# An attention and two feed-forward layers on one core: the order of softmax steps, key sums and weight splits in the front is changed

## The reference

```python
# q, k, v: (4, 8, 576, 64); factor = 4; scale = 1 / sqrt(64)
q_d, k_d, v_d = (mean of 4 neighbouring positions of q, k, v)      # 144 positions
out_d = softmax(scale * q_d @ k_d.T) @ v_d                         # "group" attention
out_up = np.repeat(out_d, 4, axis=2)
mask = np.abs(pos[:, None] - pos[None, :]) < 4                     # "local" attention
out_local = softmax(where(mask, scale * q @ k.T, -1e9)) @ v
x = (out_up + out_local) as 2304 tokens x 512
h = x @ w_in                                # 512 -> 1024
solu = h * softmax(h)
x = layer_norm(solu) * g_ln @ w_out         # 1024 -> 512
h = x @ w_in2                               # 512 -> 2048
y = (h * cos(h)) @ w_out2                   # 2048 -> 512
```

## Time and profile before

| | us |
|---|---|
| median of 3 runs | 724.93 (724.43 to 725.05) |
| the profiled execution | 727.04 |
| its span, first to last instruction | 725.3 |
| mean granted clock of TensorE | 0.993 of full speed |
| busy: TensorE, VectorE, ScalarE, GpSimd | 710.7, 393.4, 358.1, 167.3 |
| `hidden(0)` starts at | 45.98 |

### The profile page before, as it was taken

One profiled execution on the slowest core, in us unless ns is written; L12 is line 12 of the kernel. 1 busy time (PEld: TensorE's weight loads), 2 busy tenths in 40 slices (PEclk: granted clock), 3 DMA queues, 4 the chain that ended last, 5 costly groups with the idle time before them and its releaser, 6 DMA issues.

```text
span 725.3 us, 12913 instructions
## 1 busy us (share of the span) xinstructions
PE 710.7 (98%) x4937; PEld 629.7 (87%) x4937; DVE 393.4 (54%) x740; ACT 358.1 (49%) x747; POOL 167.3 (23%) x261
## 2 busy tenths in 40 slices
PE   7889999999999999999999999999999999999998
PEld 4567889889889898999989989989989989989986
DVE  5779974664562232329785464445444544554462
ACT  3567874655564544627654343434344343434343
POOL 6876764453521212100010010001000100100010
PEclk9899999999999999999999999999999999999999
DMA  8833322231106200300001000100010010001001
GB/s 295 305 111 113 104 73 72 90 124 46 53 2 253 96 0 1 117 1 0 1 1 45 1 0 1 45 0 1 1 44 0 1 43 0 0 0 43 0 0 43
DMA packets 10180, 38.63 MB, mean 53 GB/s; under 512 B 1296, under 2 KB 1296, under 8 KB 9488
## 3 DMA queue, kind: packets, MB, share of 16 engines
q1 hardware_dynamic: 10128, 37.92, 14.9%
HBM read 33.20 MB, written 4.72 MB: 52 GB/s over the span
## 4 chain that ended last, share of the span: by engine, by line
PE 94%; DVE 3%; issue 1%; POOL 1%; ACT 1%; POOLq 0%; ACTq 0%
PE ps L1179 28%; PE ps L1194 28%; PE ps L1075 14%; PE ps L1106 14%; PE ps L1090 2%; PE ps L990 2%; PE ps L1052 1%; PE ps L1038 1%; PE ps L1027 1%; PE ps L1002 1%; PE ps L983 1%; DVE xT L824 1%; PE ps L1012 1%; DVE w_split L834 1%; PE ps L1114 1%
## 5 line engine op out<-in xcount | busy, mean ns | idle before, releaser
L1179 PE MATMUL ps<-y_hi,wi 128*128 128x384 f32 x768 | 212.2, 337 | 0.0
L1179 PEld LDWEIGHTS ps<-y_hi,wi 128*128 128x128 f32 x768 | 140.4, 188 | 4.4 <-issue 0.3
L939 DVE TENSOR_SCALAR whole<-turn 128x384 f32<-128x384 f32 x96 | 45.9, 478 | 159.6 <-ACT turn L729 159.5
L1179 PE MATMUL ps<-y_lo,wi 128*128 128x384 f32 x384 | 128.9, 336 | 0.0
L729 ACT ACTIVATE turn<-ps,quarter 128x384 f32<-128x384 f32 x96 | 55.5, 579 | 144.7 <-PE ps L1179 144.7
L1194 PE MATMUL ps<-wo_hi,g_lo 128*128 128x512 f32 x288 | 113.9, 396 | 0.0
L1194 PE MATMUL ps<-wo_lo,g_hi 128*128 128x512 f32 x288 | 113.7, 395 | 0.0
L524 POOL TENSOR_TENSOR y_lo<-xT,y_hi 128x1536 fp32r<-128x1536 f32 x7 | 24.6, 3510 | 379.8 <-ACT y_hi L650 379.8
L1194 PE MATMUL ps<-wo_hi,g_hi 128*128 128x512 f32 x288 | 111.9, 389 | 0.0
L1106 PE MATMUL ps<-ln_hi,w_split 128*128 128x384 f32 x384 | 102.1, 339 | 0.0
L734 ACT ACTIVATE turn<-turn 128x384 f32<-128x384 f32 x96 | 50.5, 526 | 74.3 <-DVE turn L942 74.3
(11 more groups left out here) (100 smaller groups left out, 959.9 us busy)
## 6 DMA issues: line engine op xcount, KB each, us to landing
qk_in<-in_qk SPq DMA_DIRECT2D x16, 586.0 KB, 4.0
vblk<-in_v_blocks SPq DMA_DIRECT2D x16, 384.0 KB, 4.7
v<-in_v_rows SPq DMA_DIRECT2D x16, 288.0 KB
result<-o_sb SPq DMA_DIRECT2D x18, 256.0 KB, 2.1
raw_i<-in_w_in SPq DMA_DIRECT2D x1, 4096.0 KB, 13.3
raw<-in_w SPq DMA_DIRECT2D x4, 512.0 KB, 6.4
raw<-in_w SPq DMA_DIRECT2D x2, 1024.0 KB, 7.6
raw_o<-in_w_out SPq DMA_DIRECT2D x1, 2048.0 KB, 7.4
```

The lines of the kernel that those rows point to most:

```text
L939: nc.vector.tensor_scalar(whole[s % 2][:], turn[s % 2][:], ROUND, -ROUND, ALU.add, ALU.add).then_inc(whole_ready, 1)
L1179: last = nc.tensor.matmul(hT_ps[s % 4], wi[:, j, w, part], x[y][:, c, :], start=(c == 0 and w == 0 and x is y_hi), stop=(c == KC - 1 and w ...
```

## The change

VectorE sums the keys of pairs 0 and 1 in one reduction over four neighbours (new `sum_k` on VectorE), and GpSimd's `sum_k` stays for pairs 2 and later. SyncE's `load_qk` waits for `k_summed` instead of `k_paired`. On VectorE `probs` is cut into `group_sums` and `local_probs`. For pair 0 the local probabilities are finished ahead of pair 1's maxima, and its transposes come in the order 0, 2, 1, 3, with `local_exp(1)` between ScalarE's copies and `group_exp(1)` behind `copy_group_out(0)`. `results(0)` waits for all four copies. The eight `warm` matmuls ahead of pair 0 go, and the two inside each round write to the other pair's bank.

In `hidden(t)` the loop over the three products is now the outer one, and the products with `in_lo` come last. The `split_in1` of the front are spread differently: on ScalarE 3, 2, 3, 0 after the pairs (before 4, 2, 2, 0), on VectorE 2, 1, 1, 4 (before 4, 1, 1, 2).

```diff
@@ -45,7 +45,6 @@
 INV_2PI = 0.15915494309189535
 TWO_PI = 6.283185005187988
 DMA = 16
-T_ORDER = (1, 3, 0, 2)
 GSCALE = D ** -0.5 / FACTOR ** 2
 FRONT = 4
 FREE = PAIRS - FRONT
@@ -79,6 +78,11 @@
 
     quarters = (KC - 1) * (t > 0) + (KC - 1) * (t > FRONT)
     return t + quarters + (c + 1 if t in (0, FRONT) else 1)
+
+
+def t_order(i):
+
+    return (1, 3, 0, 2) if i else (0, 2, 1, 3)
 
 
 def before_in_banks(i):
@@ -322,7 +326,7 @@
                 n = i % 2
                 need(sp, scores_ready, i - 1)
                 need(sp, q_paired, i - 1)
-                need(sp, k_paired, i - 1)
+                need(sp, k_summed, i - 1)
                 sp.dma_start(qk_in[n][:], qk[i]).then_inc(qk_loaded[n], DMA)
 
             def load_v4(i):
@@ -415,7 +419,7 @@
                 need(pool, k_summed, i)
                 src = qk_in[n][:, 1, PAD:PAD + S].rearrange("p (g r) -> p g r", r=2)
                 nc.gpsimd.tensor_tensor(pairs_k[:], src[:, :, 0], src[:, :, 1], ALU.add).then_inc(k_paired, 1)
-                pool.wait_ge(k_paired, i + 1)
+                pool.wait_ge(k_paired, i - 1)
                 need(pool, gscores_ready, i - 1)
                 two = pairs_k[:].rearrange("p (g r) -> p g r", r=2)
                 nc.gpsimd.tensor_tensor(kgT[n][:], two[:, :, 0], two[:, :, 1], ALU.add).then_inc(k_summed, 1)
@@ -486,9 +490,8 @@
             nc.gpsimd.memset(minus_half[:], -0.5).then_inc(consts_set, 1)
 
             sum_q(0)
-            sum_k(0)
             sum_q(1)
-            sum_k(1)
+            pool.wait_ge(q_summed, 4)
             sum_v(0)
             group_probs(0)
             for i in range(FRONT):
@@ -552,7 +555,7 @@
                                          accum_out=soft[n][0:2 * GQ, 13 + x:14 + x]).then_inc(gexp_ready, 1)
 
             def copy_probsT(i, x):
-                act.wait_ge(prT_ready, 4 * i + T_ORDER.index(x) + 1)
+                act.wait_ge(prT_ready, 4 * i + t_order(i).index(x) + 1)
                 if x in (0, 2):
                     need(act, out_ready, i)
                 else:
@@ -651,18 +654,21 @@
 
             act.wait_ge(quarter_set, 1)
             nc.scalar.activation(dummy[:, 0:1], quarter[:], ACT.Exp)
-            for i in range(2):
-                local_exp(i)
-                group_exp(i)
+            local_exp(0)
+            group_exp(0)
             for i in range(FRONT):
-                for x in T_ORDER:
+                for x in t_order(i):
                     copy_probsT(i, x)
+                    if i == 0 and x == 2:
+                        local_exp(1)
                 copy_group_out(i)
+                if i == 0:
+                    group_exp(1)
                 if i:
                     local_exp(i + 1)
                     group_exp(i + 1)
                 split_quarter(0, i)
-                for c in ((0, 1, 2, 3), (4, 5), (6, 7), ())[i]:
+                for c in ((0, 1, 2), (3, 4), (5, 6, 7), ())[i]:
                     split_in1(c)
 
             for t in range(TILES):
@@ -794,7 +800,13 @@
                 dve.wait_ge(gscores_ready, i + 1)
                 nc.vector.tensor_reduce(gstat_ps(i, 0), g_ps(i), AX_X, ALU.max).then_inc(gmax_ready, 1)
 
-            def probs(i):
+            def sum_k(i):
+                n = i % 2
+                dve.wait_ge(qk_loaded[n], DMA * (i // 2 + 1))
+                src = qk_in[n][:, 1, PAD:PAD + S].rearrange("p (g r) -> p g r", r=FACTOR)
+                nc.vector.tensor_reduce(kgT[n][:], src, AX_X, ALU.add).then_inc(k_summed, 1)
+
+            def group_sums(i):
                 n = i % 2
                 dve.wait_ge(gexp_ready, 3 * i + 3)
                 nc.vector.tensor_scalar(gstat_ps(i, 1), soft[n][0:2 * GQ, gsum], SM_EPS, float(FACTOR), ALU.add,
@@ -802,6 +814,9 @@
                 dve.wait_ge(gsum_steps, 2 * i + 1)
                 need(dve, gprobs_ready, i - 1)
                 nc.vector.reciprocal(soft[n][0:2 * GQ, ginv], gstat_ps(i, 1)).then_inc(gsum_steps, 1)
+
+            def local_probs(i):
+                n = i % 2
                 e = pr[n][:].rearrange("p b s k -> p (b s) k")
                 dve.wait_ge(exp_ready, i + 1)
                 nc.vector.tensor_reduce(sums_ps(i), e, AX_X, ALU.add).then_inc(sum_steps, 1)
@@ -812,6 +827,10 @@
                 dve.wait_ge(sum_steps, 3 * i + 3)
                 nc.vector.tensor_tensor(e, e, inverses_ps(i).unsqueeze(2).broadcast_to([P, 2 * SLOTS, KEYS]),
                                         ALU.mult).then_inc(probs_ready, 1)
+
+            def probs(i):
+                group_sums(i)
+                local_probs(i)
 
             def add_scales(i):
                 dve.wait_ge(out_ready, i + 1)
@@ -880,11 +899,16 @@
             past = S + PAD - (NBLK - 1) * BLK
             nc.vector.memset(band_bf[KEYS:P, SLOTS - 1, past:KEYS], MASKED).then_inc(band_steps, 1)
 
-            for i in range(2):
-                local_shift(i)
-                group_max(i)
-            probs(0)
-            probs(1)
+            sum_k(0)
+            local_shift(0)
+            sum_k(1)
+            group_max(0)
+            local_probs(0)
+            group_sums(0)
+            local_shift(1)
+            group_max(1)
+            local_probs(1)
+            group_sums(1)
             for i in range(FRONT):
                 add_scales(i)
                 if 0 < i < FRONT - 1:
@@ -892,7 +916,7 @@
                 if i + 2 <= FRONT:
                     group_max(i + 2)
                     local_shift(i + 2)
-                for c in ((0, 1, 2, 3), (4,), (5,), (6, 7))[i]:
+                for c in ((0, 1), (2,), (3,), (4, 5, 6, 7))[i]:
                     split_in1(c)
 
             for t in range(TILES):
@@ -1032,7 +1056,7 @@
             def results(i):
                 n = i % 2
                 pe.wait_ge(v_summed, i + 1)
-                pe.wait_ge(prT_copied, 4 * i + 2)
+                pe.wait_ge(prT_copied, 4 * i + (2 if i else 4))
                 for h in range(2):
                     for c in range(2):
                         last = nc.tensor.matmul(o_ps_pair(i, 2, 0, G)[h * D:(h + 1) * D, :],
@@ -1065,16 +1089,21 @@
                     pe.wait_ge(out_added, 3 * PAIRS)
                 else:
                     pe.wait_ge(u_ready, t - 1)
-                for c in range(KC):
-                    pe.wait_ge(x_hi_ready, x_parts(t, c))
-                    pe.wait_ge(x_lo_ready, x_parts(t, c))
-                    if t == 0:
-                        pe.wait_ge(w1_ready[0], 2 * c + 2)
-                    for x, w in ((x_hi, in_hi), (x_hi, in_lo), (x_lo, in_hi)):
+                for x, w in ((x_hi, in_hi), (x_lo, in_hi), (x_hi, in_lo)):
+                    for c in range(KC):
+                        if w is in_lo:
+                            if t == 0:
+                                pe.wait_ge(w1_ready[0], 2 * c + 2)
+                        elif x is x_lo:
+                            pe.wait_ge(x_lo_ready, x_parts(t, c))
+                        else:
+                            pe.wait_ge(x_hi_ready, x_parts(t, c))
+                            if t == 0:
+                                pe.wait_ge(raw1_split[0], 2 * c + 2)
                         for f in range(2):
                             last = nc.tensor.matmul(h_ps(t)[:, f, :], x[n][:, c, :], w[:, 2 * c + f, :],
                                                     start=(c == 0 and x is x_hi and w is in_hi),
-                                                    stop=(c == KC - 1 and x is x_lo))
+                                                    stop=(c == KC - 1 and w is in_lo))
                 last.then_inc(h_ready, 1)
 
             def transpose_ln(t, half):
@@ -1120,13 +1149,13 @@
             for i in range(2):
                 scores(i)
                 group_scores(i)
-            keep_busy(0, 8)
             for i in range(FRONT):
-                transpose_probs(i, 1)
-                transpose_probs(i, 3)
-                keep_busy(i, 2)
-                transpose_probs(i, 0)
-                transpose_probs(i, 2)
+                a, b, c, d = t_order(i)
+                transpose_probs(i, a)
+                transpose_probs(i, b)
+                keep_busy(i + 1, 2)
+                transpose_probs(i, c)
+                transpose_probs(i, d)
                 keep_busy(i + 1, 4)
                 results(i)
                 if i + 2 <= FRONT:
```

## The result

The changed kernel takes 725.98 us in the median (19 runs, 725.11 to 727.93). The kernel before takes 724.33 (19 runs, 722.27 to 727.0). The ratio is 1.0027 with a 95% interval of 1.0017 to 1.0037: 1.2 to 2.7 us slower. The forecast was 724.8, with 0.1 us less or no change as the likeliest. The measured median lies within the stated range of 722.7 to 727.1, but it moved the other way, and clear of its interval. The two profiled executions say the opposite: 727.04 with a span of 725.3 before, 726.21 with a span of 724.4 after. That contradiction is the subject of this study.

What follows compares the result with a forecast made beforehand. TensorE, busy 710.7 of 725.3 us, was taken as the bound, with gains only in the front's idle and half-clock stretches. S -0.3, clock in pair 0 +0.5 and tile 0 -0.3 gave -0.1, so 724.8 from 724.93; range 722.7 to 727.1.

Steps and rivals of the forecast that it cites:

- S: Start of `hidden(0)` on TensorE: 45.98 in the profile before, 45.7 forecast, 0.3 us sooner.
- the old half-clock round: Pair 2's round, R1 to R2, in the profile before: 11.2 us, partly at half clock; forecast to be gone.
- R1: End of `results(1)` on TensorE: 26.05 in the profile before, 29.6 forecast (30.9 if the clock returns late).
- R0: End of `results(0)` on TensorE: 19.08 in the profile before, 16.55 forecast, 2.5 us sooner.
- Splits: The two `split_in1` on VectorE before `add_scales(1)`: 1.1 us each, ending at 29.1, just inside R1.
- R2: End of `results(2)` on TensorE: 37.28 in the profile before, 37.0 forecast.
- R3: End of `results(3)` on TensorE: 44.69 in the profile before, 44.4 forecast.
- Clock in pair 0: Without the eight `warm` matmuls the clock may fall about 11.6, delaying `results(0)` by 0.95 or 0 us; +0.5 taken.
- Tile 0: `split_out1` run beside POOL's q and k sums, ahead of `add_scales(4)` and `scores(5)`: 0 to -0.7 us, -0.3 taken.
- SP's queue: Load order on SP; `load_qk(4)` lands at 34.1, just ahead of need: no cost taken, up to 0.5 us in the range.
- Rival 1: Clock returns late after the long hole (6.3 us half speed) or stays low into round 2: 725.4 to 726.5; chance 0.25.
- Rival 2: The hole costs no clock fall, or pair 2's q and k sums are quicker: 722.4 to 722.9; chance 0.15.

Runs made afterwards that it cites:

- e6_softmax_only: The changed kernel with the weight splits and the product order in `hidden(t)` as before: 726.12 us, ratio 1.0024 to the kernel before.
- e2_sums_first: The changed kernel with GpSimd's product of pair 1 moved behind the q and k sums of pair 2: 723.92 us, ratio 0.9992 to the kernel before.
- e3_warm_hole: The changed kernel with 22 matmuls on the constant tile behind `results(0)`, filling the hole: 723.84 us, ratio 0.9995 to the kernel before.
- e4_splits_only: The kernel before with only the change's spread of `split_in1` and its product order in `hidden(t)`: 722.45 us, ratio 0.9982.
- e13_order_only: The kernel before with only the change's new product order in `hidden(t)`: 724.47 us, ratio 1.0000.

## Why the prediction was wrong

**The step that failed** is the one that turned the sum into a time: "The profiled execution took 727.04 ... The runs shown have the median 724.93, 2.1 under it; the same difference gives 724.8." The difference between two profiled executions was laid on the median as if 2.1 us were a constant. It isn't one. Most of it was half-clock time that this one execution had and most others have not: S was 1.3 to 2.9 us sooner in the three other profiles, and only 4 of 110 executions have a mean clock as low as its 0.993. With it, "the old half-clock round" was booked as something that the change takes away (6.8 us at half clock after R1), where the three others have 3.4 there. By an estimate from the profiles, S lies between 43.3 and 44.3 in a median execution of before (724.33 less 681.06 or 680.01), not at 45.98, and between 44.5 and 45.8 in one of the changed kernel (725.98 less 681.47 or 680.18). There most of the 1.65 us should be: time less S has the same mean in both kernels' profiles within 0.2 us. Between the profiled executions the change gained 0.83 us where 0.1 was forecast, so better terms laid on the same baseline would have missed by more, with 724.1. The warning stood in the numbers given: the profiled execution was 2 us above all three runs shown, and I noted it and did not ask what made it so.

**Point by point, against the changed kernel's first profile:**

- `sum_k(0)`: 0.72 forecast, 0.75 measured. R0: 16.55 forecast, 16.91 measured. Right; the 0.36 come from the start, where the scores of pair 0 ran until 7.0 and took 1.34 us, where they took 0.81 in before's first profile.
- `group_exp(1)` behind `copy_group_out(0)`, POOL's product and sums behind it, `group_scores(2)` at 21.8: measured 17.68, 18.16 and 22.02, with a hole of 5.1 us. Right, and it is the loss: filled or shortened, it gives back 2.3 to 2.5 us.
- The clock falls in the hole: right. It came back 5.3 us after work began again (4.1 in the second profile), between the 3.6 that I took and the 6.3 that I kept for the rival (6.6 by the slice 35 to 36 of the earlier trace rows: 0.73 is half clock to 35.54). R1: 29.6 forecast, 30.50 measured.
- Splits "at 1.1 each ... end at 29.1, just inside R1": 1.45 each, and they ended at 30.12, still inside.
- R2, R3 and S: 37.0, 44.4 and 45.7 forecast; 37.64, 45.04 and 46.03 measured. Rounds of 7.1 and 7.4 us, as forecast.
- Clock in pair 0, +0.5: no fall there in the five profiles with this order and nothing filled in before R0 (the changed kernel twice, `e6_softmax_only`, `e2_sums_first`, `e3_warm_hole`). The term was 0.
- Tile 0, -0.3: in the profile `scores(5)` starts 9.6 after S, where it was 10.56; the term was -0.96, because `split_out1` took 1.83 and not 2.79. Against the median it is less, since two other profiles of before had 1.58 and 2.42 for it.
- `hidden(0)` with no wait inside: true in the first profile, untrue in the second (1.09).
- SP's queue: no cost in these two profiles for pair 4, but pair 5's load was late in the second.

So the order of events was forecast within 1.0 us up to S, against the wrong baseline. Rival 1, the clock back late, is near to what the profile shows, and it too was added to 724.93 as though before's slow stretches were in that number. Rival 2 did not occur: the clock fell in both profiles of the changed kernel, and all 19 of its timed executions have a mean clock of 0.995 or less.

## What to carry to other kernels

Before a difference to a profiled execution is laid on a median, compare that execution's own time with the median, and say which rows hold the excess; here it was a stretch at half clock that comes in some executions only, and booking it as a gain turned a loss of 1.65 us into "no change". When work is moved ahead on one engine, follow each later engine's queue to the next thing that TensorE waits for: pair 0 came 2.2 us sooner, and a product queued ahead of the next pair's sums turned that into 5 us of standing still. Where a short hole before dense work can't be removed, a few matmuls that nobody reads are cheap: eight of them gave 1.2 us. And where each execution's mean clock is on record, sort the times by it before comparing medians.

## What the runs showed of the hardware

The moment at which the clock falls or returns is not tied to the program: in four executions of one kernel the fall after the same hole came at 28.7, 29.1, 29.2 and 27.9, once for 6.8 us and three times for 3.4 (the hole ended at 28.98, 29.32, 28.04 and 27.99), and the hole of 1.4 to 2.0 us before `group_scores(0)` was followed by a fall in two and by none in two. In `e4_splits_only` and `e13_order_only` it fell at 12.5 and 12.7, just after a hole of 2.2 and 2.3 us before `group_scores(1)`, for 3.4 us each. In or just after a hole of 5.1 us it fell in all three profiles that have one, each time for 6.8 us. The Trainium skill, "TensorE: Matmul & The Clock Gate", section "What's actually happening", says that the monitor runs free of the kernel's start; the trace agrees, by the moments just given. Here the clock makes the larger part of the spread between executions of before: their medians go from 722.9 to 726.0 us with the mean clock.

The granted clock of the windows misses the start. In the changed kernel's first profile it reads 1.00 from 5.0 to 7.0, yet the mask and products of `scores(0)` took 0.74 and 1.34 us there; in its second they took 0.44 and 0.81, as they do later at full clock. 0.74 is what the mask takes at half clock (9.20 in before's first profile). By these lengths the moment of full speed at the start differs between executions too, and that is not in the half-clock times above. The rows of the first profile:

```profile
5.00 0.74 PE L1007 MATMUL ps<-band_bf,ident_bf 128*128 128x320 bf16 x2
5.67 1.34 PE L1014 MATMUL ps<-qk_in 64*64 64x64 f32 x40
```

VectorE's weight splits and GpSimd's v sums take longer where they overlap, and which of them pays differs from place to place. In the changed kernel's timeline the two splits from 27.22 took 1.45 each, and the second v sum beside them 1.05 instead of 0.72; the single split at 43.78 took 0.68, and the first v sum beside it 1.81 instead of 1.27:

```profile
28.52 1.05 POOL L435 TENSOR_TENSOR vsums<-vpairs 72x256 f32<-72x256 f32 x1
...
43.78 0.68 DVE L853 TENSOR_TENSOR w_split<-raw,w_split 128x512 fp32r<-128x512 f32 x1
...
43.78 1.81 POOL L431 TENSOR_TENSOR vpairs<-v 72x512 f32<-72x512 f32 x1
```

The reductions `sum_k(0)` and `sum_k(1)` beside GpSimd's q sums took 0.75 and 0.74, and the q sums kept their 0.67 and 0.92.
